# Reordering a stage's loads, lowered weights and the split of x in a fused attention and feed-forward kernel

## The reference

```python
for t in range(S):                                   # attention
    kt, vt, rt, wt = (k[:, :, t], v[:, :, t], r[:, :, t], w[:, :, t])
    cur = np.einsum('bhd,bhe->bhde', u[None] * kt, vt)
    y[:, :, t] = np.einsum('bhd,bhde->bhe', rt, state + cur)
    state = wt[:, :, :, None] * state + np.einsum('bhd,bhe->bhde', kt, vt)
...
rms = np.sqrt(np.mean(x * x, axis=-1, keepdims=True) + 1e-06)     # gated layer
xn = x / rms * rms_g
g = xn @ w_gate
x = g * (1.0 / (1.0 + np.exp(-g))) * (xn @ w_val) @ w_out
...
r = np.maximum(x @ w_in, 0.0)                        # squared layer
out = (s * (r * r) + b) @ w_out
```

## Time and profile before

| | |
|---|---|
| three runs | 1032.35, 1033.99, 1034.6 us; median 1033.99 us |
| profiled execution | 1030.35 us, its span 1028.2 us (2.1 us lie around the span) |
| TensorE busy | 1000.8 us, 97% of the span |
| VectorE, ScalarE, GpSimd busy | 527.7, 331.5 and 266.6 us |
| granted TensorE clock, mean | 0.997 of 2.4 GHz |

### The profile page before, as it was taken

One profiled execution on the slowest core, in us unless ns is written; L12 is line 12 of the kernel. 1 busy time (PEld: TensorE's weight loads), 2 busy tenths in 40 slices (PEclk: granted clock), 3 DMA queues, 4 the chain that ended last, 5 costly groups with the idle time before them and its releaser, 6 DMA issues.

```text
span 1028.2 us, 24563 instructions
## 1 busy us (share of the span) xinstructions
PE 1000.8 (97%) x10614; PEld 867.1 (84%) x10614; DVE 527.7 (51%) x700; ACT 331.5 (32%) x563; POOL 266.6 (26%) x189
## 2 busy tenths in 40 slices
PE   5989989999999999999999999999999999999998
PEld 5868878887888888888888887898998989989888
DVE  6889936772676377647752224605317044061350
ACT  1442323132322322331323444505326044161340
POOL 4655722561255145415620460000000000000000
PEclk9999999999999999999999999999999999999999
DMA  7380240033013201410103411001010010100000
GB/s 267 117 323 3 99 149 32 3 136 113 33 48 129 74 33 48 165 67 3 48 3 129 148 31 62 1 24 39 9 54 0 23 38 8 54 0 15 15 8 23
DMA packets 21978, 66.12 MB, mean 64 GB/s; under 512 B 2944, under 2 KB 6272, under 8 KB 20608
## 3 DMA queue, kind: packets, MB, share of 16 engines
q1 hardware_dynamic: 21312, 63.65, 17.4%
q10 hardware_dynamic: 576, 1.13, 0.3%
HBM read 55.34 MB, written 9.44 MB: 63 GB/s over the span
## 4 chain that ended last, share of the span: by engine, by line
PE 95%; DMA 2%; DVE 2%; issue 1%; ACT 0%; SPq 0%; ACTq 0%; DVEq 0%
PE o_ps L567 15%; PE o_ps L1312 15%; PE value_ps L555 14%; PE gate_ps L555 14%; PE level_ps L45 10%; PE level_ps L427 5%; PE mix_ps L1312 5%; PE gate_ps L45 5%; PE value_ps L45 5%; PE level_ps L501 2%; PE mix_ps L501 2%; PE level_ps L479 1%; DMA arena<-wT 1%; DMA masks<-c_masks 1%; PE level_ps L443 1%
## 5 line engine op out<-in xcount | busy, mean ns | idle before, releaser
L1386 DVE SCALAR_TENSOR_TENSOR sqr<-relu,sb_col 128x512 f32<-128x512 f32 x96 | 72.2, 752 | 217.4 <-ACT relu L1344 217.4
L1105 POOL TENSOR_TENSOR R<-R,arena 128x512 f32<-128x512 f32 x72 | 115.3, 1619 | 198.1 <-PE level_ps L427 177.0
L976 DVE TENSOR_TENSOR u_raw<-value_ps,u_raw 128x512 f32<-128x512 f32 x66 | 45.5, 690 | 123.6 <-PE value_ps L555 123.6
L749 ACT ACTIVATE u_raw<-gate_ps 128x512 f32<-128x512 f32 x72 | 43.0, 598 | 185.0 <-PE gate_ps L555 185.0
L1312 PE MATMUL o_ps<-wt_hi,g_lo 128*128 128x384 f32 x288 | 96.2, 334 | 0.0
L1312 PE MATMUL o_ps<-wt_hi,g_hi 128*128 128x384 f32 x288 | 96.2, 334 | 0.0
L1312 PE MATMUL o_ps<-wt_lo,g_hi 128*128 128x384 f32 x288 | 96.2, 334 | 0.0
L756 ACT ACTIVATE u_hi<-u_raw 128x512 fp32r<-128x512 f32 x66 | 41.7, 631 | 147.3 <-DVE u_raw L976 147.3
L567 PE MATMUL o_ps<-u_hi,wo_hi 128*128 128x512 f32 x216 | 88.9, 411 | 0.0
L555 PE MATMUL value_ps<-x_hi,w_hi 128*128 128x512 f32 x216 | 85.6, 396 | 2.3 <-DVE u_raw L976 2.3
L567 PE MATMUL o_ps<-u_hi,wo_lo 128*128 128x512 f32 x216 | 85.2, 395 | 0.0
(11 more groups left out here) (167 smaller groups left out, 2139.2 us busy)
## 6 DMA issues: line engine op xcount, KB each, us to landing
kr_nat<-kr SPq DMA_DIRECT2D x10, 1152.0 KB, 5.2
K<-kT SPq DMA_DIRECT2D x12, 512.0 KB, 6.9
arena<-wT SPq DMA_DIRECT2D x12, 512.0 KB, 7.7
R<-rT SPq DMA_DIRECT2D x10, 512.0 KB, 3.9
w_raw<-wgv SPq DMA_DIRECT2D x12, 384.0 KB, 5.6
v_sb<-v SPq DMA_DIRECT2D x12, 384.0 KB, 4.8
x_scratch<-x_sb SPq DMA_DIRECT2D x18, 256.0 KB, 2.3
x_raw<-x_scratch SPq DMA_DIRECT2D x6, 768.0 KB, 4.4
```

Of the source, the lines that this page charges most:

```text
L749: act.activation(u[:, f % 2], gate_ps[:], ACT.Silu).then_inc(silu_done, 1)
L976: dve.tensor_tensor(u[:, f % 2], value_ps[:], u[:, f % 2], ALU.mult).then_inc(u_done, 1)
L1105: pool.tensor_tensor(q, q, decay(blk, l, 0), ALU.mult).then_inc(rmul_done, 1)
L1386: dve.scalar_tensor_tensor(out=sq[f % 2][:], in0=relu[f % 2][:], scalar=sb_col[:, 0:1], in1=relu[f % 2][:], op0=ALU.mult, op1=ALU.mult).th ...
```

## The change

Three edits; the two tables of numbers belong to the second:

1. The loads of a stage. Before, the natural tile of the next stage stood ahead of the keys, and decays ahead of queries and values. Now the keys come first; queries and values of block 0 and both decays stand behind the first reading; queries and values of block 1 and the natural tile behind the second. In stage 0 the keys no longer wait for `y_done`, and the values go behind all weights.
2. Three lowered weight pieces (`lower_out_weights(0)`, `lower_weights(2)`, `lower_weights(3)`) and the keys' product of level 0 move from ahead of the first product of u to behind it; other pieces move by a few groups.
3. At the passage `x_hi` and `x_lo` of the first superblock are made in three parts (one for each 128 channels), and TensorE waits for each part where it uses it.

```diff
-LATE_WEIGHTS = (2, 8, 11, 14, 17, 20, 23, 25)
-LATE_OUT = (5, 10, 16, 21, 27)
+LATE_WEIGHTS = (5, 7, 9, 11, 14, 17, 20, 23, 28)
+LATE_OUT = (8, 13, 16, 21, 27)
...
+        for blk in range(2):
+            load_keys(1, blk)
         sp.wait_ge(y_done, 2)
         for blk in range(2):
-            load_keys(1, blk)
+            load_decay(1, blk)
             load_queries(1, blk)
-        for blk in range(2):
-            load_decay(1, blk)
...
-        load_values(1, 0)
-        load_values(1, 1)
         for f in range(9, F1):
             load_weights(f)
             load_out_weights(f - 6)
+        load_values(1, 0)
+        load_values(1, 1)
...
             if s + 1 < NSB:
-                load_natural(2 * s + 2)
                 for blk in range(2):
                     load_keys(s + 1, blk)
+                load_queries(s + 1, 0)
+                load_values(s + 1, 0)
                 for blk in range(2):
                     load_decay(s + 1, blk)
-                for blk in range(2):
-                    load_queries(s + 1, blk)
-                    load_values(s + 1, blk)
+                load_queries(s + 1, 1)
+                load_values(s + 1, 1)
+                load_natural(2 * s + 2)
...
-        act.activation(x_hi[:], x_raw[:], ACT.Copy).then_inc(xhi_done, 1)
+        for k in range(KT):
+            act.activation(x_hi[:, k], x_raw[:, k], ACT.Copy).then_inc(xhi_done, 1)
...
             if k == 0 and s == 1:
                 decays_after(s, 0)
+            if k == 1 and s == 1:
                 keys_after(s, 0)
-            if k == 1:
+                lower_out_weights(0)
+            if k == (2 if s == 1 else 1):
                 decays_after(s, 1)
+            if k == 3 and s == 1:
+                lower_weights(2)
...
             if s == 1 and k in LATE_WEIGHTS:
-                lower_weights(4 + LATE_WEIGHTS.index(k))
+                lower_weights(3 + LATE_WEIGHTS.index(k))
...
-            lower_out_weights(0)
-            lower_weights(2)
-            lower_weights(3)
...
-        wait(dve, xhi_done, split_tiles(NSB - 1, KT - 1) + 1)
-        dve.tensor_tensor(x_lo[:], x_raw[:], x_hi[:].bitcast(F32), ALU.subtract).then_inc(xlo_done, 1)
+        lower_x(NSB)
...
+    def first_x_ready(eng, k):
+        wait(eng, xlo_done, split_tiles(NSB, k))
...
+                    hidden_tile(pe, h_ps[f % HB], f, win_hi, win_lo, x_hi, x_lo,
+                                first_x_ready if first and f == 0 else None).then_inc(h_done[0], 1)
```

More of the change, by code:

```diff
@@ L37, with hidden_tile @@
 NSB = NTOK // T
-def hidden_tile(pe, ps, f, win_hi, win_lo, x_hi, x_lo):
+def hidden_tile(pe, ps, f, win_hi, win_lo, x_hi, x_lo, x_ready=None):
     for k in range(KT):
+        if x_ready:
+            x_ready(pe, k)
         cols = slice(k * FF2 + f * P, k * FF2 + (f + 1) * P)
@@ L646, in _ @@
                     attention(s, k)
-        wait(pe, xlo_done, split_tiles(NSB - 1, KT - 1) + 1)
         wait(pe, winlo_done, NBLK)
@@ L1198, in _ @@
                 lower_wt(k // 3 - 2)
-    return win_hi, win_lo, wt_hi, wt_lo, sb_col, x1_done
+    def first_x_ready(eng, k):
+        wait(eng, xlo_done, split_tiles(NSB, k))
+    return win_hi, win_lo, wt_hi, wt_lo, sb_col, x1_done, first_x_ready
 class Counters:
@@ L1225, in squared_phase @@
 def squared_phase(nc, block, a, x1_dram, x1_out, out, x_hi, x_lo, win_hi, win_lo, wt_hi, wt_lo, sb_col, x1_done,
-                  const_in, h_ps, out_ps):
+                  first_x_ready, const_in, h_ps, out_ps):
     with ExitStack() as ctx:
@@ L1301, in body @@
                         await_step(pe, relu_done, n, f - HB + 1)
-                    hidden_tile(pe, h_ps[f % HB], f, win_hi, win_lo, x_hi, x_lo).then_inc(h_done[0], 1)
+                    hidden_tile(pe, h_ps[f % HB], f, win_hi, win_lo, x_hi, x_lo,
+                                first_x_ready if first and f == 0 else None).then_inc(h_done[0], 1)
                 for t in range(TT):
```

## The result

| | before | after |
|---|---|---|
| median of the runs | 1034.30 us (4 runs, 1032.35 to 1036.43) | 1021.42 us (4 runs, 1021.07 to 1021.90) |
| profiled execution, span | 1030.35, 1028.2 us | 1021.45, 1019.3 us |
| mean granted clock of it | 0.997 | 1.0 |

The ratio is 0.9875, with a 95% interval of 0.9855 to 0.9895: the change makes the kernel faster by 1.05 to 1.45%.

What follows compares the result with a forecast made beforehand. TensorE, busy 1000.8 of 1028.2 us, was taken as the bound, leaving only idle time and clock. Terms 2.33 + 4.31 + 1.54 + 0.81 = 8.99 us took 1033.99 to 1025.0 us; range 1022.5 to 1030.5 us.

Steps and rivals of the forecast that it cites:

- first product of u: Second value tile of stage 1: TensorE's 2.33 us wait for VectorE's product goes, with 1.3 us margin.
- VectorE's debt: Rival: moved work delays the state, so stage 1's first reading waits up to 2.25 us; chance 0.09 for over 1 us.
- hole of stage 1: Reading of stage 1, from 132.00 us: the 2.66 us "issue" hole closes; up to 0.3 us may stay.
- half clock behind it: Out tile behind stage 1's hole: without that stop no half clock, 3.81 to 2.27 us, 1.54 us won.
- hole of stage 2: Reading of stage 2, from 233.30 us: the 1.65 us "issue" hole closes; up to 0.3 us may stay.
- passage: Start of the squared phase: the wait for `x_lo` goes, gain 0.81 us, lower bound 0.28 us.
- I carry the difference over: Last step: the shown runs' median stays 3.64 us above the profiled execution, so 1033.99 - 9.0 = 1025.0 us.
- longer holes: Unprofiled runs may have longer holes than the profiled one; the range takes in another 2 us below for it.
- The packet of instructions: Readings of stages 1 and 2: TensorE's 16 KB instruction packet stood behind load data; emptier engines close both holes, 4.31 us.
- next packet behind the new loads: Rival: second reading's packet falls behind loads issued after the first, hole up to 2.9 us; chance 0.12 for one or two stages.
- Slower: Rival: late next packet in all four stages, with half clock each time, 17.8 us lost against 9.0 won: 1042.8 us; chance 0.05.
- The holes are not the loads': Rival: the readings' holes and half clock stay, gain only 2.33 + 0.81, 1030.8 us; chance 0.06.

Runs made afterwards that it cites:

- the repeat: The kernel before, unchanged, run once more: 1033.34 us, ratio 0.9993, profiled 1034.31 us.
- the shifted stream: The kernel before with 25 small unused matmuls (100 TensorE instructions) added in a pause of stage 0, loads untouched: 1028.80 us, ratio 0.9965.
- the longer stops put in: The changed kernel with a TensorE stop in each of stages 1 to 5, made by 21 small unread ScalarE copies: 1042.62 us.

## Why the prediction was wrong

**Own execution: right.** 1021.3 us forecast, 1021.45 measured, and the mechanism of each term was there. That the total is so close is in part luck: what the entry gave and the state's wait took, both put at nothing, cancel. Their sizes (measured is how much TensorE's lead over the trace before grew):

| term | forecast | measured |
|---|---|---|
| first product of u | 2.33 | 2.72, from 0.55 to 3.27 us ahead |
| entry | 0 | 0.55 |
| VectorE's debt | 0 (0 to 2.25) | -0.52 |
| hole of stage 1 | 2.66 (a rest up to 0.3) | 2.15 (rest 0.53) |
| half clock behind it | 1.54 | 1.49 |
| hole of stage 2 | 1.65 (a rest up to 0.3) | 1.33 (rest 0.43 on the trace) |
| passage | 0.81 | 1.09 |
| sum | 8.99 | 8.81 |

The entry is all up to the first gate tile of stage 1: a wait 1.1 us shorter and no half clock, against the two new waits of 0.7 us. The readings' rests passed their bound of 0.3 us a little: the packet needs 2.4 us even with empty engines, as the prediction took from loaded ones, but it began 1.0 us into the reading and the instructions in hand lasted 2.8 us. The debt was smaller than its upper bound and not nothing: VectorE took up 2.8 us of it where it had been waiting (busy 32.50 against 29.73 us), yet the moved work grew on the way. The second level's first key product took 1.81 us beside GpSimd's query products at 69.28 us, where two took 1.29 us without them.

By the Trainium skill (SBUF — State Buffer, "two separate sides") an operation of VectorE with two inputs from SBUF, as these have, and GpSimd take turns for a whole instruction. The trace agrees in both directions: the two decays took 3.94 us before with GpSimd beside them and 1.44 us now nearly without. The moved pieces, for which the prediction feared it, did not fall beside GpSimd (`wo_lo` 0.95 us, as before).

**The step that failed: "The median of the runs shown is 3.64 us above that execution; I carry the difference over."** The difference is not a constant around the kernel. The changed kernel's median lies 0.03 us from its profiled execution (0.25 us over ten runs), and that is the whole of the miss. The 3.64 us came apart so:

- 1.1 us is that the three runs shown had a median of 1033.99 us, above the 1032.87 us of 101 runs.
- 1.7 us is half clock. The profiled run before had two stretches, its plain runs have 3.3 on average, and the 27 with two stretches have a mean of 1031.19 us. In the change's ten runs there are 0.4. So for the medians the clock was worth about 2.9 x 1.44 = 4.2 us, where the sum had one stretch, 1.54 us, and the pair of profiled runs two.
- 0.8 us, by which the profiled run lies below those 27, stays open; holes of stage 0 that differ from run to run are a candidate, not shown.

The prediction did widen the range downwards by 2 us, but for "longer holes" in unprofiled runs; the repeat rejects that for the readings (2.65 and 1.70 us), and the right reason would have asked for more.

That a stop can bring half clock by itself is shown, by stops of 2.6 us with idle queues (4.3 stretches a run) against stops of 1.5 us (0.9). It is not the only way to it, as the three stretches of the shifted stream show. Why it falls to one execution and not to the other is open. Of the stops of the kernel before, the change removes one (2.33 us) and shortens three: 2.66 to 0.53 and 1.65 to 0.43 in readings, 2.71 to 1.59 at the entry. By the table of stops two of these four are of a length that nearly always brings half clock, and the other two sometimes.

**The packet of instructions: right, and shown** by the shifted stream, which moved the holes without moving a load. The rivals: *next packet behind the new loads* did not come in stages 1 to 4, but narrowly: the packet of the second reading began at 131.2 us, and the new loads, issued from 130.53 us on, moved their first data at 131.5 us. It came in stage 0, 0.66 us at 47.03 us behind the early keys, a place where the prediction had looked at landing times only. *VectorE's debt* came with 0.6 us. *Slower* did not. *The holes are not the loads'* is out.

By the Trainium skill (Runtime: NRT & Kernel Launch, "Instruction fetch mechanics") the fetch of the next 16 KiB block is mostly hidden. The block size agrees (16 KB a packet; up to the last one, at 744 us, 18343 of TensorE's matmuls and weight loads in 73 packets, about 250 for each); the hiding fails in readings, by 0.4 to 0.8 us with empty engines and by up to 3.8 us with full ones.

**The edits together.** Loads alone 7.6 us, passage 1.2, and what is left of 11.2 (1032.87 - 1021.70, the median of ten runs), 2.4 us, falls to the product of u, though alone it won nothing. The 1.2 us and so the 2.4 us are no surer than the runs: by the traces they are 1.1 and 2.7. The prediction added its terms as if each stood alone; its sum holds only for all three edits together.

## What to carry to other kernels

- A median and a profiled execution may differ by states inside the kernel, not around it. Take the mean granted clock of every run, count the stretches, and price a stop with its likely share of a 1.5 us stretch (here nearly one for 2.6 us and more, about a fifth for 1.5 to 2.4 us), not with what one trace shows behind it.
- Where TensorE is sent many small instructions in a row, keep the DMA engines empty as that part begins; one transfer of 1.1 MB a stage, moved from ahead of it to behind it, was worth 5.8 us here.
- Freeing one engine pays only when what it then waits for comes earlier as well: the same edit won nothing alone and about 2.4 us behind the moved loads.

## What the runs showed of the hardware that I had not expected

- A packet of TensorE's instructions is used 2.4 us after it begins, with empty engines (127.39 to 129.76 us) as with full ones (132.27 to 134.66), and 2.2 to 2.8 us in the readings of the other traces: what full engines delay is its beginning.
- 100 extra instructions of no use made the kernel before some 4 us faster (1028.80 against 1032.87 us), mainly because packet borders moved away from the readings.
- Stops of TensorE of 2.6 us and more were followed by half clock in 15 of 16 cases in the traces, those of 1.5 to 1.9 us inside readings in 4 of 10, and those of 1.5 to 1.75 us elsewhere in none of 15; behind the longer stops put in the half clock came with a DMA share of 0.00.
- Half clock also came without a stop: three stretches in a row beside small matmuls, from 59.0 us on in the trace of the shifted stream.
